# A branch prefetch hint at the top of TensorE's loop over rounds

## The chip, the cores and the metric

The kernel runs on one core of one Trainium2 chip. The metric is the device time of one execution in microseconds. Three executions of the kernel before gave 1239.11, 1243.03 and 1248.18 us, so the median is 1243.03 us.

## The reference

The inputs are float32: `x` of 4 x 4096 x 192, `weight_gen` of 4 x 4096 x 8 x 7, `w_in` of 192 x 2048 and `w_out` of 2048 x 192. What is computed is a dynamic causal convolution over seven taps, followed by a gated two-layer product on all 16384 tokens:

```python
w = exp(weight_gen - max(weight_gen, axis=-1))        # softmax over the 7 taps
w = w / (sum(w, axis=-1) + 1e-09)
out = einsum('bshk,bskhg->bshg', w, x_unf)            # x_unf: the 7 latest tokens, zeros before the start
x = out.reshape(16384, 192)
h = x @ w_in
g = h * clip(h + 3.0, 0.0, 6.0) / 6.0
return g @ w_out
```

## The kernel before, in words

The work is cut into 16 rounds (`PAIRS`) of 1024 tokens. A round has two halves of 512 tokens. GpSimd computes the convolution of each half (`attend`), TensorE transposes it, and then 16 tiles of 128 hidden columns are filled: TensorE computes `h` of a tile into one of four PSUM banks (`work`), ScalarE takes relu(h + 3) (L261), VectorE multiplies (L357), ScalarE rounds the product to the type that the matmuls read (`g_hi`, L266), VectorE stores what the rounding lost (`g_lo`, L362), and TensorE multiplies both parts by `w_out` into four PSUM banks `sums` (L548 and L551). The float32 precision is kept by products of such high and low parts, which is why there are many matmuls per tile.

TensorE works on two tiles at a time, a duo. In a round there are 18 duos, 16 of tiles and 2 of transposes. One duo is: a wait until VectorE has left the banks (`bank_free`), the first half of the fill (L512 and L513), a few products of earlier tiles, the second half of the fill (L526 and L527), and products again. The Python loop over the 18 duos is written out, and only the loop over rounds is a loop on the chip. It runs 15 times on TensorE, and the sixteenth round is written out behind it. So one iteration is one long piece of straight code: 856 matmuls, each with its weight load, and 88 instructions that count registers, wait or branch, 1800 in all. Its last instruction is a compare-and-branch back to its first. The branch is taken 14 times; the fifteenth time it falls through to the last round.

The other engines have loops over rounds of their own (SyncE, GpSimd, ScalarE and VectorE), each far shorter than TensorE's: 14 rows of instructions on SyncE, 47 on GpSimd, 121 on ScalarE and 136 on VectorE. The engines meet only through semaphores, and the order of work on each is written out by hand in the program; no scheduler moves anything.

All instructions that the loop itself makes (the register of the round, its increase, and the branch) have the line of the `with` statement, L586. The first matmul of an iteration is that of L512 for duo 3, the last ones are L548 and L551 of duo 20.

Of the kernel before, what the change touches and what calls it, by code (L numbers as in the profile page):

```python
# [26 lines left out]
PAIRS = S // (RUNS * TOKENS)  # L27
# [419 lines left out]
def tensor_program(nc, pe, t, s):  # L447
# [110 lines left out]
    def duo(q, d, last=False):  # L558
        bank_free(q, 2 * d - 3, last)
        fill_first(q, d, last)  # L560
        starts = d % HALF_DUOS == FIRST_DUO
        multiply(q, parts_after(d, 0), 1, None if starts else turns_before(q, d, 0), by_sets=starts)
        fill_second(q, d, last)
        multiply(q, parts_after(d, 1), 0, turns_before(q, d, 1))
# [18 lines left out]
    multiply(0, parts_after(FIRST_DUO, 1), 0, 2)  # L583
    pe.wait_ge(s.w_out_lo, 2)

    with pe.Fori(0, PAIRS - 1) as q:  # L586
        for d in range(FIRST_DUO + 1, FIRST_DUO + 1 + DUOS):
            duo(q, d)
    for d in range(FIRST_DUO + 1, DUOS + 2):
# [89 lines left out]
def build(nc, *arrays):  # L679
    with ExitStack() as ctx:  # L680
        dram = Dram(*arrays)
        t = Buffers(lambda name, shape, dt=F32: ctx.enter_context(nc.sbuf_tensor(name, shape, dt)),
                    lambda name, shape: ctx.enter_context(nc.psum_tensor(name, shape, F32)))
        s = Semaphores(lambda name: ctx.enter_context(nc.semaphore(name)))
        block = ctx.enter_context(nc.Block())

        @block.sync
        def _(sp):
            sync_program(nc, sp, dram, t, s)

        @block.gpsimd
        def _(pool):
            gpsimd_program(nc, pool, t, s)

        @block.scalar
        def _(act):
            scalar_program(nc, act, dram, t, s)

        @block.vector
        def _(dve):  # L700
            vector_program(nc, dve, t, s)

        @block.tensor
        def _(pe):
            tensor_program(nc, pe, t, s)
# [17 lines left out]
```

## Time and profile before

| | |
|---|---|
| median of three executions | 1243.03 us |
| profiled execution | 1239.38 us |
| its span, from the first to the last instruction | 1236.6 us |
| mean granted TensorE clock | 0.985 of full speed |
| TensorE busy with matmuls | 1170.4 us, 95% of the span |
| VectorE, ScalarE, GpSimd busy | 66%, 54%, 56% |
| instruction fetches (queue q8) | 139 packets, 2.28 MB |

### The profile page before, as it was taken

To read this page: it belongs to the slowest core of one execution; us is meant where nothing else is said; L and a number is where in the kernel's file an instruction comes from. 1 tells how busy PE (TensorE), PEld (TensorE's weight loads), DVE (VectorE), ACT (ScalarE), POOL (GpSimd) and SP (SyncE) were. 2 spreads that over 40 slices of the span, in tenths; PEclk is the share of its full clock that TensorE was granted. 3 is DMA by queue.
4 is the path that set the end of the run, shared out by engine and by line. 5 is a ranking of instruction groups with operands and counts; after the bars stand their busy time and mean duration, and the time that the engine had idled before them with its cause. 6 is when DMAs were issued, how large, how long until landed. Compare 5 with 4: busy or idle time off the path is not lost.

```text
span 1236.6 us, 33823 instructions
## 1 busy us (share of the span) xinstructions
PE 1170.4 (95%) x13696; PEld 1095.7 (89%) x13696; DVE 818.9 (66%) x1362; ACT 662.4 (54%) x1269; POOL 691.1 (56%) x455
## 2 busy tenths in 40 slices
PE   1999999999999999999999999999999999999998
PEld 1898998989989898998989989899898989989997
DVE  7866766657666666666667666676666666666664
ACT  3554555545555455455555555555454555555553
POOL 7793671927639085490936719276390854909300
PEclk9999999999999999999999999999999999999999
DMA  6101010010100101001010100101001010010000
GB/s 177 46 22 59 20 48 15 22 60 21 47 15 22 60 22 59 2 29 52 22 60 16 52 15 22 60 22 58 3 22 60 22 59 2 27 54 14 15 15 14
DMA packets 12203, 44.25 MB, mean 36 GB/s; under 512 B 1183, under 2 KB 5279, under 8 KB 10139
## 3 DMA queue, kind: packets, MB, share of 16 engines
q1 hardware_dynamic: 12059, 41.93, 9.7%
q8 instruction: 139, 2.28, 0.8%
q14 instruction: 5, 0.04, 0.0%
HBM read 29.34 MB, written 12.58 MB: 34 GB/s over the span
## 4 chain that ended last, share of the span: by engine, by line
PE 92%; DVE 3%; ACT 2%; issue 1%; POOL 1%; DMA 0%; DVEq 0%; ACTq 0%
PE sums L548 32%; PE work L512 16%; PE work L526 13%; PE sums L551 13%; PE work L527 9%; PE work L513 7%; DVE g_lo L362 2%; DVE work L357 1%; ACT g_hi L266 1%; ACT relu L261 1%; PE work L477 1%; PE work L464 1%; POOL pool_acc L166 0%; POOL pool_prod L164 0%; DVE w_in L413 0%
## 5 line engine op out<-in xcount | busy, mean ns | idle before, releaser
L548 PE MATMUL sums<-w_out,g_hi 64*128 64x384 f32 x4096 | 649.7, 357 | 2.8 <-DVE g_lo L362 2.1
L551 PE MATMUL sums<-w_out,g_lo 64*128 64x192 f32 x4096 | 558.4, 249 | 0.0
L357 DVE SCALAR_TENSOR_TENSOR work<-relu,work 128x512 f32<-128x512 f32 x512 | 331.2, 693 | 331.1 <-ACT relu L261 329.8
L261 ACT ACTIVATE relu<-work 128x512 f32<-128x512 f32 x512 | 279.4, 601 | 400.6 <-PE work L527 398.2
L548 PEld LDWEIGHTS sums<-w_out,g_hi 64*128 64x128 f32 x4096 | 438.4, 186 | 19.8 <-issue 3.1
L551 PEld LDWEIGHTS sums<-w_out,g_lo 64*128 64x128 f32 x4096 | 442.9, 189 | 0.2
L266 ACT CAST g_hi<-work 128x512 fp32r<-128x512 f32 x512 | 300.9, 588 | 76.0 <-DVE work L357 73.6
L362 DVE TENSOR_TENSOR g_lo<-work,g_hi 128x512 fp32r<-128x512 f32 x512 | 330.1, 687 | 14.4
L159 POOL TENSOR_TENSOR pool_acc<-x_in,w_soft 128x768 f32<-128x768 f32 (+1 forms) x32 | 50.0, 1562 | 461.4 <-DVE w_soft L351 454.6
L166 POOL TENSOR_TENSOR pool_acc<-pool_acc,pool_prod 128x768 f32<-128x768 f32 (+1 forms) x160 | 295.6, 1847 | 0.0
L512 PE MATMUL work<-xt_a,w_in 64*128 64x512 f32 x768 | 235.7, 414 | 35.9 <-DVE g_lo L362 28.1
L164 POOL TENSOR_TENSOR pool_prod<-x_in,w_soft 128x768 f32<-128x768 f32 (+1 forms) x160 | 248.6, 1554 | 0.0
L513 PE MATMUL work<-xt_a,w_in 64*128 64x512 f32 x768 | 235.4, 413 | 0.0
L526 PE MATMUL work<-xt_a,w_in 64*128 64x512 f32 x768 | 226.8, 401 | 0.0
L527 PE MATMUL work<-xt_a,w_in 64*128 64x512 f32 x768 | 226.4, 401 | 0.0
L512 PEld LDWEIGHTS work<-xt_a,w_in 64*128 64x128 f32 x768 | 126.1, 190 | 51.0 <-DVE g_lo L362 33.5
L512 PE MATMUL work<-xt_b,w_in 64*128 64x512 f32 (+1 forms) x512 | 133.0, 340 | 0.0
L513 PE MATMUL work<-xt_b,w_in 64*128 64x512 f32 (+1 forms) x512 | 132.9, 340 | 0.0
L526 PE MATMUL work<-xt_b,w_in 64*128 64x512 f32 (+1 forms) x512 | 129.3, 332 | 0.0
L527 PE MATMUL work<-xt_b,w_in 64*128 64x512 f32 (+1 forms) x512 | 129.2, 332 | 0.0
L526 PEld LDWEIGHTS work<-xt_a,w_in 64*128 64x128 f32 x768 | 124.1, 187 | 5.4
L513 PEld LDWEIGHTS work<-xt_a,w_in 64*128 64x128 f32 x768 | 126.2, 190 | 1.4
(47 smaller groups left out, 960.4 us busy)
## 6 DMA issues: line engine op xcount, KB each, us to landing
x_in<-x_dram SPq DMA_DIRECT2D x15, 1344.0 KB, 6.0
out_dram<-out_stage SPq DMA_DIRECT2D x32, 384.0 KB, 3.0
w_raw<-weight_gen_dram SPq DMA_DIRECT2D x16, 224.0 KB, 3.0
w_out_raw<-moe_w_out_dram SPq DMA_DIRECT2D x1, 1152.0 KB, 13.3
x_in<-x_dram SPq DMA_DIRECT2D x1, 768.0 KB, 5.0
w_in_raw<-moe_w_in_dram SPq DMA_DIRECT2D x1, 768.0 KB, 8.1
w_in_raw<-moe_w_in_dram SPq DMA_DIRECT2D x2, 384.0 KB, 10.1
w_out_raw<-moe_w_out_dram SPq DMA_DIRECT2D x1, 384.0 KB, 6.2
```

The lines of the kernel that those rows point to most:

```text
L164: eng.tensor_tensor(prod[k % 3], x_tap(k), w_tap(k), ALU.mult).then_inc(step, 1)
L166: eng.tensor_tensor(acc, acc, prod[(k - 1) % 3], ALU.add).then_inc(step, 1)
L261: nc.scalar.activation(t.relu[:, m % 2, :], t.work[m % BANKS][:], ACT.Relu, bias=3.0).then_inc(s.relu_ready, 1)
L266: nc.scalar.copy(t.g_hi[:, m % G_SLOTS, :], t.work[m % BANKS][:]).then_inc(s.g_hi_ready, 1)
L357: nc.vector.scalar_tensor_tensor(bank[:], t.relu[:, m % 2, :], 6.0, bank[:], ALU.min, ALU.mult).then_inc(s.gated, 1)
L362: nc.vector.tensor_tensor(t.g_lo[:, m % G_SLOTS, :], t.work[m % BANKS][:], f32(t.g_hi[:, m % G_SLOTS, :]), ALU.subtract).then_inc(s.g_lo_r ...
L512: nc.tensor.matmul(*upper, start=(i == 0), stop=False)
L513: ins = nc.tensor.matmul(*lower, start=(i == 0), stop=False)
L526: ins_upper = nc.tensor.matmul(*upper, start=False, stop=(i == len(both) - 1))
L527: ins_lower = nc.tensor.matmul(*lower, start=False, stop=(i == len(both) - 1))
L548: nc.tensor.matmul(t.sums[n][:, 0:2 * D], t.g_hi[rows, m % G_SLOTS, n * P:(n + 1) * P], t.w_out[rows, j, :], start=(j == 0 and part == 0), ...
L551: ins = nc.tensor.matmul(t.sums[n][:, D:2 * D], t.g_lo[rows, m % G_SLOTS, n * P:(n + 1) * P], t.w_out[rows, j, 0:D], start=False, stop=las ...
```

## The change

One line is different. The loop over rounds on TensorE is opened by the general form, for that engine alone, with the option `hint_back_edge`:

```diff
-    with pe.Fori(0, PAIRS - 1) as q:
+    with nc.Fori(0, PAIRS - 1, engines=[mybir.EngineType.PE], hint_back_edge=True) as q:
         for d in range(FIRST_DUO + 1, FIRST_DUO + 1 + DUOS):
             duo(q, d)
```

In the program this adds one instruction to TensorE's stream. It stands first in the loop's body, so it is executed in each of the 15 iterations, and it names the compare-and-branch at the end of the body, with the outcome "likely taken". The piece of the difference on TensorE at the loop's entry, behind the products ahead of the loop:

```order
 L551 MATMUL sums<-w_out,g_lo 128x192 x2
 L586 UNCONDITIONAL_BRANCH
+L586 BRANCH_PREFETCH_HINT
 L586 ISA
 L512 MATMUL work<-xt_a,w_in 128x512
```

The unconditional branch leads into the loop, the hint is new, and the row "ISA" is the register work that was the first instruction of the body before. The other end of the body, on TensorE too, reads as before:

```order
L551 MATMUL sums2<-w_out,g_lo 128x192
L551 MATMUL sums3<-w_out,g_lo 128x192
L586 REGISTER_ALU
L586 COMPARE_AND_BRANCH
L512 MATMUL work2<-xt_a,w_in 128x512
L513 MATMUL work3<-xt_a,w_in 128x512
```

The compare-and-branch is the instruction that the hint names. The matmuls behind it are the first of the sixteenth round. Nothing is moved, and the other four engines' programs are the same.

## Rows read from the trace of the kernel before

**Rows 1.** The page: span, busy times, queue of instruction fetches (packets, MB, share).
```profile
span 1236.6 us, 33823 instructions
PE 1170.4 (95%) x13696; PEld 1095.7 (89%) x13696; DVE 818.9 (66%) x1362; ACT 662.4 (54%) x1269; POOL 691.1 (56%) x455
q8 instruction: 139, 2.28, 0.8%
```

**Rows 2.** Waits of PE, whole span: us in total, times, longest us.
```profile
PE work L512 <- DVE g_lo L362: 28.1, 12, 2.6
PE work L463 <- POOL attn_b L170: 22.9, 1, 22.9
PE work L512 <- issue: 5.4, 2, 2.7
PE work L512 <- DVE xt_b L371: 2.4, 1, 2.4
PE sums L548 <- DVE g_lo L362: 2.1, 1, 2.1
```

**Rows 3.** Stretches between two iterations: window, us, busy per engine, PEclk, DMA share, GB/s.
```profile
114.68:117.42 2.74, 0.00 (x1) 0.01 (x1) 2.65 (x5) 0.92 (x2) 0.00 (x0) 1.00 0.02 7
...
342.33:344.33 2.00, 0.01 (x1) 0.01 (x1) 1.95 (x4) 0.91 (x2) 0.00 (x0) 1.00 0.00 0
...
1091.92:1094.59 2.67, 0.01 (x2) 0.01 (x1) 2.58 (x5) 0.90 (x2) 0.00 (x0) 0.99 0.02 7
sum 33.46, PE 0.04 PEld 0.09 DVE 32.27 ACT 12.66 POOL 0.00; mean PE 0.00 PEld 0.01 DVE 2.31 ACT 0.90 POOL 0.00
```

**Rows 4.** Instructions of L586: count, ns least/median/most, first and last start.
```profile
L586 PEldq FUSED_REGOPS  x15: 50/50/53, 41.7 to 1094.5; - x15
L586 PEldq COMPARE_BRANCH  x15: 83/3582/4007, 113.2 to 1166.6; - x15
```

**Rows 5.** Same columns: iterations at full clock, six in all, first and last.
```profile
42.75:114.68 71.93, 71.92 (x860) 66.38 (x856) 50.58 (x85) 41.15 (x80) 52.20 (x35) 1.00 0.15 54
...
1019.92:1091.92 72.00, 72.00 (x856) 67.71 (x856) 47.48 (x82) 39.99 (x78) 43.14 (x28) 1.00 0.10 35
sum 431.33, PE 431.31 PEld 403.52 DVE 287.88 ACT 241.13 POOL 267.85; mean PE 71.88 PEld 67.25 DVE 47.98 ACT 40.19 POOL 44.64
```

**Rows 6.** Same columns: eight iterations partly at lower clock, first and last.
```profile
117.42:190.71 73.29, 73.28 (x856) 68.04 (x856) 46.94 (x81) 40.01 (x78) 43.12 (x28) 0.98 0.10 35
...
944.78:1017.78 73.00, 73.00 (x856) 68.65 (x856) 47.33 (x81) 40.02 (x78) 43.12 (x28) 0.98 0.10 35
sum 587.05, PE 587.02 PEld 548.87 DVE 377.53 ACT 320.01 POOL 345.02; mean PE 73.38 PEld 68.61 DVE 47.19 ACT 40.00 POOL 43.13
```

**Rows 7.** Same columns: the fifteenth iteration's stretch.
```profile
1094.59:1166.50 71.91, 71.91 (x838) 68.17 (x840) 45.50 (x79) 38.75 (x76) 43.15 (x28) 0.98 0.03 12
```

**Rows 8.** Timeline of DVE, at the loop's entry and at one edge: start, us.
```profile
40.84 1.29 DVE L362 TENSOR_TENSOR g_lo<-work,g_hi 128x512 fp32r<-128x512 f32 x2
...
188.38 1.29 DVE L362 TENSOR_TENSOR g_lo<-work,g_hi 128x512 fp32r<-128x512 f32 x2
189.70 1.29 DVE L357 SCALAR_TENSOR_TENSOR work<-relu,work 128x512 f32<-128x512 f32 x2
191.05 1.29 DVE L362 TENSOR_TENSOR g_lo<-work,g_hi 128x512 fp32r<-128x512 f32 x2
```

**Rows 9.** DMA over 192.91:268.63, one iteration with its edge: packets, MB.
```profile
q8 instruction: 9, 0.15, 0.9%
```

**Rows 10.** DMA over 186:194 in 40 slices of 0.2 us: GB/s, fetch packets.
```profile
GB/s 0 0 0 0 0 0 0 0 0 0 0 82 215 399 399 338 399 108 0 15 97 15 31 31 0 0 0 0 0 0 0 0 0 0 0 0 0 0 0 82
q8 instruction: 3, 0.05, 2.5%
```

## The prediction

> **What bounds the kernel now.** I read the page first. The span is 1236.6 us and TensorE is busy for 1170.4 us of it, 95%; the next engine, VectorE, has 818.9 us [rows 1]. So TensorE sets the time, and only its idle time and its speed can change. Next I read its waits [rows 2]. One of 22.9 us is the start, before the first transposes. The rest is nearly all one group: before L512, 28.1 us in 12 waits and 5.4 us in 2 waits, 14 waits of up to 2.7 us each. Fourteen is the number of times the loop over rounds goes back to its top. The stretches between iterations show that these waits are all there: 14 of them, 33.46 us in sum, 2.39 us each, with TensorE at nothing and GpSimd at nothing [rows 3].
>
> The view puts 12 of these waits down to VectorE's `g_lo`. That must be checked, because a hint to the branch can't help a wait for data. Across the edge from 190.71 to 192.91 us, VectorE ends a pair of `g_lo` at 188.38 + 1.29 = 189.67 us and the next pair only at 192.34 us [rows 8]. The fill at the top of an iteration writes the banks of two duos earlier, so it needs the first pair, and that was over 3.2 us before TensorE went on and 1.0 us before it stopped. The later pair is what `g_lo` happened to end in the gap. What did hold TensorE stands in the rows of L586: the compare-and-branch took 83 ns at its shortest, which is the one that fell through, and 3582 ns in the median and 4007 ns at most [rows 4]. A taken branch is thus some 3.5 us dearer than one not taken. The sequencer reaches it ahead of the matmuls: the first branch starts at about 113.2 us [rows 4], the last matmul ends at 114.68 us [rows 3]. So about 1.4 us of it is covered, and the remainder is the gap.
>
> What the branch does in that time is seen in the instruction queue. One iteration fetches 9 packets of about 16 KB (0.15 MB) [rows 9], and the whole run 139 [rows 1]. Around one edge, a single packet in a slice of 0.2 us reads as 82 GB/s: one at 188.2 to 188.4 us, one at 190.0 to 190.2 us (97, with 15 of other traffic) and one at 193.8 to 194.0 us [rows 10]. The branch was reached shortly before the second. I read this as follows: the first packet is the code behind the branch, fetched in advance and not used; the second is the top of the loop, fetched only when the branch asks for it; the third is the block after it.
>
> Last, the clock. Six iterations ran wholly at the granted clock of 1.00 (2.4 GHz) and took 71.88 us in the mean (431.33 / 6) [rows 5]. Eight show a mean of 0.98, part of them at the lower level, and took 73.38 us (587.05 / 8) [rows 6]; the fifteenth shows 0.98 too [rows 7]. The first iteration was entered without an edge and has 1.00. Of the 14 behind a gap nine show 0.98 and five 1.00. I read the fall as something that a gap brings about in some cases: 1.50 us each.
>
> **The change, part by part.** It adds one instruction at the top of the body and names the branch at its end as likely taken. Nothing else moves.
>
> *The gaps.* If the top of the loop is at hand when the branch is taken, the branch costs what the untaken one does, 83 ns, which lies within the 1.4 us by which the sequencer is ahead. Then the whole 33.5 us goes.
>
> *The clock.* Without gaps, the nine iterations at 73.38 us become like the six at 71.88 us: 9 x 1.50 = 13.5 us. The lower end of this term is 0 (the clock falls for another reason), the upper 13.5 us. I take 13.5, since the only iteration without a gap before it had none.
>
> *What is late next.* The gap let the other engines catch up, so their margin must be looked at. The first iteration has none of it: VectorE's pair of `g_lo` ends at 40.84 + 1.29 = 42.13 us [rows 8], and the first fill starts at 42.75 us [rows 5]. That is 0.6 us of margin, and that iteration took 71.93 us with the softmax work of the next round in it, no longer than the others at full clock. No wait takes the gap's place. GpSimd works 43 to 52 us in an iteration of 72 us [rows 5], ScalarE 40, VectorE 48.
>
> *The hint itself.* No row shows one. The nearest are the 50 ns of the register operation beside it and the 83 ns of the untaken branch [rows 4]. Hidden behind the queued matmuls it costs 0; fully exposed, 15 x 0.083 = 1.2 us. I take 0, because the sequencer is ahead at this place.
>
> *The exit.* The fifteenth time the branch falls through. If the hint brings the top of the loop in place of the code behind the branch, that code is missing once, when the sixteenth round comes to it. Bounds: 0, or one gap with the lower clock behind it, 2.4 + 1.5 = 3.9 us. I take 2.4.
>
> *Sum.* Against the profiled execution's 1239.4 us: 1239.4 - 33.5 - 13.5 + 2.4 = 1194.8 us. The profiled execution stands at the lower end of the three runs (1239.1 to 1248.2), 3.7 us under their median of 1243.0. Between 9 and 14 edges with the lower clock lie 7.5 us, which could be that spread, and it would go with the edges; a part may stay. I put the median after at 1196 us.
>
> *A rule against it.* The rows show that a body of 1800 instructions is fetched anew in each iteration [rows 9]. The Trainium skill ("Runtime: NRT & Kernel Launch", "Instruction fetch mechanics") says that TensorE's instruction memory is 128 KiB, or 2048 instructions, and in a note just below that it is only two lines and that prefetch is purely sequential, a taken branch out of the two lines forcing a fetch. By the 2048 instructions alone this body would fit and the edges would be free, so the trace speaks against that figure as it stands, unless the packet fetched past the branch pushes the top out. By "purely sequential" a hint could do nothing, and the sum would be 1239.4 us.
>
> **The rivals.**
>
> *A, the forecast: no gap is left.* The top of the loop is at hand at the branch. 1190 to 1199 us. Chance 0.46.
>
> *B: the fetch starts earlier, but not early enough.* The hint turns the first packet of the edge into the top of the loop. It starts 1.8 us before the one that the branch asks for now [rows 10]. Of 2.39 us, 0.6 us are left, 14 x 0.6 = 8.3 us. With no fall of the clock that gives 1194.8 + 8.3 = 1203 us; with all nine, 1216.6 us. For it speaks that in the trace of before every iteration fetches all its blocks, one at a time and just ahead of their use; against it, that one block fewer may let the whole body stay. Chance 0.33. The Trainium skill's note on two lines, on the same page, would make this case the rule, since the top lies seven lines back at the branch.
>
> *C: the hint does nothing.* Prefetching stays sequential, the branch still asks for its own target, and the time is that of before plus at most 1.2 us: 1239 to 1244 us. For it speaks that the trace of before shows sequential fetches alone. Chance 0.14. The skill's "purely sequential" is this case.
>
 The gain per iteration is (33.5 + 13.5) / 15 = 3.1 us, so one such block takes back most of it and from the second on the kernel is slower: with two 1192.4 + 15 x 2 x 2.4 = 1264 us, with all seven 1444 us. Nothing in the profile speaks for or against it. Chance 0.07.
>
> **How the numbers follow.** The predicted time is A's, 1196 us. A and B hold 0.79 and reach from 1190 us (no cost at the exit, and a little less of the rest) to 1216 us (B with the clock's falls kept), which is the range. A measurement of this kernel can tell about 1% from no change, 12 us; A and B are faster by more, 0.79; C is within it, 0.14; D is slower, 0.07.
>
> **What would show it.** In the changed kernel's profile, under A the compare-and-branch at L586 has a median near the 83 ns, the waits of L512 are gone, every iteration from the second takes about 71.9 us with a PEclk of 1.00, and the nine packets per iteration become eight or fewer; if the body stays in the memory, the run's packets fall from 139 to some 20. Under B the branch takes about 1.7 us and 14 short gaps remain, with eight packets per iteration. Under C the rows of L586 are as before, under D waits "issue" appear within the iterations. A branch that is short while gaps remain at the top would prove me wrong on VectorE: then the `g_lo` wait was real.

## The result, and the profile after

The changed kernel takes 1187.8 us in the median of four runs (1186.15 to 1189.66), against 1244.03 us of the kernel before in the runs beside it (1239.11 to 1248.18). The ratio is 0.955 with an interval of 0.9511 to 0.9588. The direction and the mechanism were those of case A, but the time lies 2.2 us under the lower end of the range (1190 us), so the range missed it. The profiled execution took 1187.49 us, 51.9 us less than that of before.

The page of the changed kernel, its span, busy times and instruction fetches:

```profile
span 1185.5 us, 33838 instructions
PE 1151.4 (97%) x13696; PEld 1070.8 (90%) x13696; DVE 818.9 (69%) x1362; ACT 662.0 (56%) x1269; POOL 690.7 (58%) x455
q8 instruction: 13, 0.21, 0.1%
```

Against [rows 1], the other engines' busy times are the same and the fetches fell from 139 packets to 13. Seven of the 13 packets come before 102 us, in the first iteration, and the next one only at 1116.6 us. So the loop's body is fetched once and then stays. Next the waits of PE in the changed kernel (us in total, times, longest), all of them:

```profile
PE work L463 <- POOL attn_b L170: 23.1, 1, 23.1
PE sums L548 <- DVE g_lo L362: 3.3, 2, 2.5
PE work L512 <- DVE xt_b L371: 2.4, 1, 2.4
PE sums L548 <- PE sums L551: 0.5, 3, 0.2
```

The 14 waits at L512 of [rows 2] are gone, also the 12 that were put down to VectorE's `g_lo`. Had they been waits for data, a hint to the branch would not have removed them. The instructions of L586 in the changed kernel (count, ns least/median/most, first and last start):

```profile
L586 PEldq BRANCH_PREFETCH_HINT  x15: 31/31/45, 41.9 to 1044.0; - x15
L586 PEldq FUSED_REGOPS  x15: 50/50/50, 42.0 to 1044.1; - x15
L586 PEldq COMPARE_BRANCH  x15: 80/216/257, 112.9 to 1115.5; - x15
```

A taken branch now takes 216 ns, not 3582 ns [rows 4], and the hint 31 ns. (The prediction had the taken branch at the 83 ns of the untaken one; both lie within the 1.4 us by which the sequencer is ahead, so nothing comes of it.) The timeline of PE in the changed kernel, across the first edge (start, us):

```profile
113.99 0.36 PE L548 MATMUL sums<-w_out,g_hi 64*128 64x384 f32 x2
114.19 0.25 PE L551 MATMUL sums<-w_out,g_lo 64*128 64x192 f32 x2
114.28 0.42 PE L512 MATMUL work<-xt_a,w_in 64*128 64x512 f32 x1
114.28 0.42 PE L513 MATMUL work<-xt_a,w_in 64*128 64x512 f32 x1
```

The next iteration's first matmuls start 0.09 us after the last one's start, as anywhere else in the stream; the last one still runs to 114.44 us. This overlap matters for the sum below.

The whole loop in one window, from the first matmul of the first iteration to the first matmul of the sixteenth round, and what follows to the end. The kernel before:

```profile
42.75:1167.83 1125.08, 1091.61 (x12844) 1021.98 (x12842) 744.48 (x1261) 613.61 (x1186) 656.01 (x427) 0.99 0.10 34
1167.83:1236.60 68.77, 63.64 (x748) 60.18 (x744) 39.21 (x66) 33.63 (x65) 0.00 (x0) 0.98 0.04 13
```

and the changed one:

```profile
42.44:1116.85 1074.41, 1074.41 (x12845) 1000.78 (x12842) 744.97 (x1262) 613.48 (x1187) 656.08 (x427) 1.00 0.09 33
1116.85:1185.50 68.65, 63.55 (x748) 58.38 (x744) 39.15 (x66) 33.54 (x65) 0.00 (x0) 0.98 0.03 13
```

The loop is 50.67 us shorter, the part ahead of it 0.31 us, the last round 0.12 us. That is the 51.1 us between the spans. Outside the span lie 0.8 us more (1239.4 - 1236.6 = 2.8 before, 1187.5 - 1185.5 = 2.0 now). An iteration takes 1074.41 / 15 = 71.63 us from start to start, TensorE is busy in all of it, and the clock is 1.00.

### The profile page after: what moved, and what is told of

It reads as the page before. It is cut to its first block, busy times and chain, and to the rows that moved or that the text cites. A ratio compares the mean times of both kernels' runs of the same rounds, so it can differ in the third digit from the quotient of the medians.

```text
span 1185.5 us, 33838 instructions
## 1 busy us (share of the span) xinstructions
PE 1151.4 (97%) x13696; PEld 1070.8 (90%) x13696; DVE 818.9 (69%) x1362; ACT 662.0 (56%) x1269; POOL 690.7 (58%) x455
## 4 chain that ended last, share of the span: by engine, by line
PE 96%; DVE 2%; POOL 1%; issue 0%; DMA 0%; ACT 0%; DVEq 0%; ACTq 0%
PE sums L548 34%; PE work L512 16%; PE sums L551 15%; PE work L526 14%; PE work L527 9%; PE work L513 7%; PE work L477 1%; PE work L464 0%; DVE w_out L419 0%; POOL pool_acc L166 0%; POOL pool_prod L164 0%; DVE w_in L413 0%; DMA w_raw<-weight_gen_dram 0%; PE work L463 0%; DVE g_lo L362 0%
## 5 line engine op out<-in xcount | busy, mean ns | idle before, releaser
L548 PE MATMUL sums<-w_out,g_hi 64*128 64x384 f32 x4096 | 631.0, 354 | 3.9 <-DVE g_lo L362 3.3
L551 PE MATMUL sums<-w_out,g_lo 64*128 64x192 f32 x4096 | 536.1, 247 | 0.0
L548 PEld LDWEIGHTS sums<-w_out,g_hi 64*128 64x128 f32 x4096 | 410.2, 184 | 23.3 <-issue 3.5
L551 PEld LDWEIGHTS sums<-w_out,g_lo 64*128 64x128 f32 x4096 | 415.7, 187 | 0.0
L512 PE MATMUL work<-xt_a,w_in 64*128 64x512 f32 x768 | 229.2, 404 | 2.4 <-DVE xt_b L371 2.4
L513 PE MATMUL work<-xt_a,w_in 64*128 64x512 f32 x768 | 229.1, 404 | 0.0
L526 PE MATMUL work<-xt_a,w_in 64*128 64x512 f32 x768 | 226.2, 400 | 0.0
L527 PE MATMUL work<-xt_a,w_in 64*128 64x512 f32 x768 | 226.1, 400 | 0.0
L512 PEld LDWEIGHTS work<-xt_a,w_in 64*128 64x128 f32 x768 | 123.6, 186 | 15.0 <-DVE g_lo L362 5.1
L512 PE MATMUL work<-xt_b,w_in 64*128 64x512 f32 (+1 forms) x512 | 129.8, 333 | 0.0
L513 PE MATMUL work<-xt_b,w_in 64*128 64x512 f32 (+1 forms) x512 | 129.7, 333 | 0.0
L526 PE MATMUL work<-xt_b,w_in 64*128 64x512 f32 (+1 forms) x512 | 129.0, 331 | 0.0
L527 PE MATMUL work<-xt_b,w_in 64*128 64x512 f32 (+1 forms) x512 | 129.0, 331 | 0.0
L526 PEld LDWEIGHTS work<-xt_a,w_in 64*128 64x128 f32 x768 | 123.3, 186 | 6.1
L527 PEld LDWEIGHTS work<-xt_a,w_in 64*128 64x128 f32 x768 | 123.3, 186 | 3.0
```

Source lines behind the costliest of these rows:

```text
L512: nc.tensor.matmul(*upper, start=(i == 0), stop=False)
L513: ins = nc.tensor.matmul(*lower, start=(i == 0), stop=False)
L526: ins_upper = nc.tensor.matmul(*upper, start=False, stop=(i == len(both) - 1))
L527: ins_lower = nc.tensor.matmul(*lower, start=False, stop=(i == len(both) - 1))
L548: nc.tensor.matmul(t.sums[n][:, 0:2 * D], t.g_hi[rows, m % G_SLOTS, n * P:(n + 1) * P], t.w_out[rows, j, :], start=(j == 0 and part == 0), ...
L551: ins = nc.tensor.matmul(t.sums[n][:, D:2 * D], t.g_lo[rows, m % G_SLOTS, n * P:(n + 1) * P], t.w_out[rows, j, 0:D], start=False, stop=las ...
```

## Experiments

The predicted rival B (an earlier fetch of the top) and the forecast A (nothing to fetch) are told apart by the packets above. Two questions were open: why the body stays, and what the lower clock hangs on. The trace suggests an answer to the first. Before, each iteration of 1800 instructions fetched nine packets of 16 KB, and one of them was the block past the branch, so the body lay in eight. Nothing was left of the top when the branch asked for it. The Trainium skill ("Advanced Engine Details and Errata", "ISA Cache") gives 256 instructions for such a block; by the runs below the tipping point agrees with that. Theory R is that TensorE's instruction memory holds eight blocks, and that the hint's effect is that this ninth block is not fetched. Rival S is that it is the hint itself that makes a far branch cheap.

**No hint, a body that lies in seven blocks or in eight.** Two kernels with the same instructions and no hint. To make the body small enough, each of the four tiles of two duos is filled without its fifth product (8 matmuls of 856 are left out); the loop's first instruction is put at place 0 or place 100 of a block.

```diff
+    def terms(d):
+        return 4 if d in (4, 5) else 5
...
-        for i, (upper, lower) in enumerate(zip(products(2 * d, 0), products(2 * d + 1, 1))):
+        for i, (upper, lower) in enumerate(zip(products(2 * d, 0)[:terms(d)], products(2 * d + 1, 1))):
...
-    with nc.Fori(0, PAIRS - 1, engines=[mybir.EngineType.PE], hint_back_edge=True) as q:
+    with nc.Fori(0, PAIRS - 1, engines=[mybir.EngineType.PE], hint_back_edge=False,
+                 head_slot={mybir.EngineType.PE: 0}) as q:
```

> No hint. Two of the 16 duos of tiles in each round fill without their fifth product, which leaves 8 matmuls of 856 out, so one iteration is 1784 instructions in place of 1800; the loop's first instruction is put at the first place of a fetched block of 256. The body then lies in 7 blocks, 8 with the one fetched past the branch. Theory R (the hint helps because the unused block behind the branch is not fetched any more, so that the whole body stays in TensorE's instruction memory, which holds 8 blocks): no gap at any edge though there is no hint, COMPARE_BRANCH about 0.2 us, some 13 to 15 instruction packets in the run, time about 1180 us (1187.8 less 16 x 0.5 us for the matmuls left out). Theory S (the hint is needed, because a taken branch far back always asks for its block again): 14 gaps of about 2.4 us, branch 3.5 us, some 125 packets, 1231 to 1238 us.

> The same instructions as the kernel whose loop starts at the first place of a block, with the same 8 matmuls of 856 left out and no hint, but the loop starts at place 100 of a block. It lies in 8 blocks, 9 with the one behind the branch. Theory R: one block too many, so every block is fetched again in each iteration: 14 gaps of about 2.4 us, 9 packets per iteration, about 139 in all, 1231 to 1238 us, some 50 us above the run with the same work. Theory S: the same as that run, whatever it gives.

Measured, one run each: 1179.09 us with the top at place 0, 1236.79 us at place 100, beside 1241.59 us of the kernel before. L589 is the loop's line here. The branch (ns least/median/most), and from the page the fetches, with the top at place 0:

```profile
L589 PEldq COMPARE_BRANCH  x16: 76/208/1495, 41.9 to 1107.8; - x16
```
```profile
q8 instruction: 14, 0.23, 0.1%
```

and the same two views with the top at place 100:

```profile
L589 PEldq COMPARE_BRANCH  x16: 83/3546/3857, 41.7 to 1164.8; - x16
```
```profile
q8 instruction: 139, 2.28, 0.7%
```

and its waits at the top:

```profile
PE work L515 <- DVE g_lo L362: 32.8, 14, 2.6
```

This decides for R. The same instructions, moved by 100 places, are 57.7 us apart, and without any hint the branch takes 0.21 us where the body and the block behind it make eight. S expected the two to be equal. (The 1495 ns are one branch at 41.9 us, the entry into the loop, which is there because of the placement.)

**Where the hint has to stand.** The loop is written out by hand, with the hint directly ahead of the closing two instructions or ahead of duo 19. Both kernels in one cut, each has one of the two marked pieces:

```diff
+        for d in range(FIRST_DUO + 1, FIRST_DUO + 1 + DUOS):
+            if d == 19:                                   # second kernel
+                place = pe.mark_branch_hint_location()
+            duo(q, d)
+        place = pe.mark_branch_hint_location()            # first kernel
+        nc.regs_alu(registers, registers, 1, op=ALU.add)
+        pe.br_lt(registers, PAIRS - 1, on_true="rounds_loop", on_false="rounds_end").branch_hint(place)
```

> All work done. The hint stands not at the top of the iteration but directly ahead of the loop's closing two instructions, 1800 instructions later, inside the block that holds the branch. If the hint acts only by steering the advance fetch that is made when the branch's block is entered (theory R), it comes too late, since that fetch is already under way: gaps of 2 to 2.6 us and about 139 packets, 1238 to 1246 us. If it makes a fetch or keeps the body by itself at whatever place it is executed (theory T), the gaps are gone or much shorter: 1188 to 1205 us.

> All work done. The hint stands ahead of duo 19, the last but one of the iteration, some 230 instructions ahead of the branch and in the block before the branch's. Theory R: as good as at the top, no gaps, 13 packets, 1186 to 1190 us. A theory by which it must be known for the whole iteration (U) gives gaps of up to 2.4 us and over 100 packets, 1200 to 1244 us.

Measured, one run each: 1251.26 us with the hint last, 5 us above the top of the expected range, and 1189.50 us with the hint ahead of duo 19. The hint, the branch, and the page's line on fetches, with the hint last:

```profile
L596 PEldq BRANCH_PREFETCH_HINT  x15: 41/41/41, 112.6 to 1179.0; - x15
```
```profile
L598 PEldq COMPARE_BRANCH  x15: 88/3578/4001, 112.8 to 1179.2; - x15
```
```profile
q8 instruction: 140, 2.29, 0.8%
```

and the same with the hint ahead of duo 19:

```profile
L594 PEldq BRANCH_PREFETCH_HINT  x15: 31/31/45, 104.1 to 1108.5; - x15
```
```profile
L598 PEldq COMPARE_BRANCH  x15: 80/216/257, 113.2 to 1117.7; - x15
```
```profile
q8 instruction: 14, 0.23, 0.1%
```

Nine microseconds ahead of the branch it does all that it does at the top, so it need not be known for the whole iteration (theory U falls). 0.2 us ahead it does nothing: in that run the packet past the branch starts at 111.8 us and the hint at 112.6 us, so that block is already on its way (theory T falls). The two kernels have the same instructions in another order, so it is neither the added instruction nor the other form of the loop that helps. These two runs alone would also fit a hint that needs some lead; the placements in nine blocks below speak for the steering of that one advance fetch. The single run of 1251.26 us was above the kernel before, and the same kernel was then timed against that one:

> All work done, the hint directly ahead of the loop's closing two instructions; timed against the kernel before. The single run of it had the old gaps and 18 stretches of half clock in place of 10. If a late hint is simply useless, the ratio to before is 0.995 to 1.005. If it costs something, 1.005 to 1.01.

Measured: 1241.35 us in the median of 10 runs against 1242.44 us of 19, a ratio of 0.9998 (0.998 to 1.0017). A late hint is useless, and no cost of it shows within 0.2%. The lines of the core in three executions, whose gaps in the loop sum to 34.7, 36.1 and 33.5 us, show where the 1251 us came from (span, mean granted clock): the kernel with the late hint, twice, and the kernel before.

```profile
core 0: 1249.5 us, clock 0.974
```
```profile
core 0: 1243.0 us, clock 0.980
```
```profile
core 0: 1236.6 us, clock 0.985
```

From 0.985 to 0.974 the time lost to the lower clock grows by an estimated 0.026 x 1249.5 - 0.015 x 1236.6 = 13.9 us, and the spans are 12.9 us apart. In the run of 1251 us the lower clock came at all 14 edges and lasted twice as long at four of them; in the kernel before it came at 9. This differs between runs of one kernel too: of the 19 runs of the kernel before, the fastest (1235.38 us) had a mean clock of 0.987 and the slowest (1244.74 us) 0.979. The 0.008 between them are an estimated 10 us, and the times are 9.4 us apart.

**A body of eight blocks or of nine, with the hint.** All work is done. Eleven increments of semaphores that nobody reads stand behind each duo. The body is then 1999 instructions long with the hint, the same in four kernels; only the place of its first instruction differs.

```diff
+    with nc.Fori(0, PAIRS - 1, engines=[mybir.EngineType.PE], hint_back_edge=True,
+                 head_slot={mybir.EngineType.PE: 30}) as q:     # 30, 50, 239, 128
         for d in range(FIRST_DUO + 1, FIRST_DUO + 1 + DUOS):
             duo(q, d)
+            for i in range(11):
+                pe.sem_inc(s.pad[i % 6], 1)
```

> All work done, hint at the top. Behind each duo stand 11 increments of semaphores that nobody reads, 198 per iteration, which makes the body 1999 instructions; the loop starts at place 30 of a block, so the body still ends in its eighth block (30 + 1999 = 2029 of 2048). Theory R (eight blocks stay): no gaps, branch 0.22 us, 13 or 14 packets, 1186 to 1192 us plus what the increments cost where the sequencer is not ahead. If they cost their 51 ns each on the path it would be 15 x 198 x 0.051 = 151 us more; I expect under 10 us, since they are spread over the duos.

> The same instructions as the kernel with the padded body in eight blocks, but the loop starts at place 50, so its branch is the very first instruction of a ninth block (50 + 1998 = 2048). Theory R: nine blocks do not stay, 9 packets per iteration, about 139 in all; the hint steers a fetch that starts only as the branch is reached, so gaps of 2 to 2.6 us, some 50 us above the eight-block run. Theory V (a hint makes the top available whatever the size of the body, by fetching it well ahead): no gaps.

> The same instructions once more, loop at place 239: the branch lies at place 189 of the ninth block (239 + 1998 = 2237). Nine packets per iteration again, but the block of the branch is entered some 7 us before the branch, more than the 3.5 us that a fetch at the branch cost. Theory R with the fetch steered on entering the block (case B of the prediction with time enough): no gaps, the time of the eight-block run, about 135 packets. If the hint only helps where the body stays: 14 gaps of 2.4 us.

> The padded instructions once more with the hint at the top (1999 per iteration), loop at place 128: nine blocks, the branch at place 78 of the ninth, and 128 instructions between the loop's first and the next block. The two other placements in nine blocks had a stall before the top (branch at place 0) or 3 us behind it (top at place 239). If one fetch at a time, each begun when a block is entered, explains both, then here both fetches are in time: about 135 packets, a branch below 1 us, no gap of over 1 us at or just behind the top, and 1277 to 1290 us, like the eight-block run. If a body that does not stay always stalls somewhere, 1325 to 1350 us.

| top at place | blocks | time, one run | branch, median | packets |
|---|---|---|---|---|
| 30 | 8 | 1277.46 us | 228 ns | 15 |
| 50, branch first in the ninth | 9 | 1348.08 us | 3344 ns | 140 |
| 239, branch at 189 of the ninth | 9 | 1329.90 us | 360 ns | 142 |
| 128, branch at 78 of the ninth | 9 | 1279.90 us | 446 ns | 141 |

The increments themselves cost 90 us against the changed kernel (1277.5 - 1187.5), where I had expected under 10: that expectation was wrong, and the comparison holds among these four alone. Twenty places further on, the body no longer stays: from 15 packets to 140, and 70.6 us more, where about 50 were expected. Eight blocks of 256 is where it tips (30 + 1999 = 2029, 50 + 1999 = 2049). The hint stood a whole iteration ahead of the branch here, and yet the packet of the top started only 1.0 us behind the branch's start, because the branch is the first instruction of its block (theory V falls). The gaps are 3.7 to 4.2 us and not 2 to 2.6: the sequencer reached this branch only as TensorE ran dry, without its lead of 1.4 us.

The kernel with its top at place 239 was expected to be as fast as the first and is not. Its timeline of PE behind one edge (start, us, idle before):

```profile
200.79 0.26 PE L551 MATMUL sums<-w_out,g_lo 64*128 64x192 f32 x2
201.82 0.49 PE L512 MATMUL work<-xt_a,w_in 64*128 64x512 f32 x1 [0.77 <-issue]
...
204.91 0.49 PE L513 MATMUL work<-xt_b,w_in 64*128 64x512 f32 x1 [1.92 <-issue]
```

and in its waits of PE there are 14 of these, 1.9 us in the mean:

```profile
PE work L513 <- issue: 26.4, 14, 2.2
```

The branch is short, but a stall ends 3 us behind the top's first matmul. The top has 17 instructions left in its own block, and the block after it is fetched only when the branch arrives at the top (its packet starts 1.1 us behind the branch's start). The stall was moved from ahead of the top to behind it. The 52.4 us over the first kernel are these 26.4 us and some 20 us of lower clock (estimated from the mean clocks, 0.983 x 1328.1 us against 0.998 x 1275.6 us); the rest was not traced.

With 128 places left, and the branch 78 places into its block, both fetches are in time. The DMA of that kernel over 192 to 200 us, in slices of 0.2 us, around the branch at 197.9 us:

```profile
GB/s 0 0 0 0 0 0 0 0 0 0 0 0 0 82 0 184 384 399 353 399 123 15 0 15 15 15 31 31 0 0 0 0 0 0 0 82 0 0 0 0
q8 instruction: 2, 0.03, 2.0%
```

The packet of the top starts 3.1 us ahead of the branch, that of the next block 1.2 us behind it; with the branch at place 189 the first starts 7.8 us ahead, with the branch at place 0 not ahead at all. So the advance fetch is tied to the entry into the branch's block, and the hint turns it to the top. 141 packets are fetched, and the kernel takes 1279.9 us all the same, 2.4 us more than the first. The earlier fetch of the top that case B of the prediction assumed exists, then, but with a body of nine blocks and not of eight.

**A gap without any fetch.** The changed kernel with increments of unread semaphores ahead of the branch, 70 of them and then 22, body in eight blocks.

```diff
             duo(q, d)
+        for i in range(22):                # 70 in the first of the two
+            pe.sem_inc(s.pad[i % 6], 1)
```

> All work done, hint at the top, body in eight blocks, so no fetches. 70 increments of unread semaphores stand directly ahead of the loop's closing instructions, 70 x 0.051 = 3.6 us of the sequencer's time, about what the taken branch took before. It makes 15 gaps of about 2.2 us with nothing fetched. If an idle TensorE alone brings the lower clock: some 7 to 14 stretches at half clock after the gaps and 1188 + 15 x 2.2 + 10 x 1.5 = about 1236 us. If the clock fell for the fetches or something else of the old edge: the clock stays at 1.00 and the time is about 1221 us.

> All work done, hint at the top, body in eight blocks, nothing fetched after the first iteration. 22 increments of unread semaphores directly ahead of the branch. By the run with 70 of them, where the gaps were 9.8 us, one costs (9.8 + 1.4) / 70 = 0.16 us of the sequencer, so 22 give 3.5 us, what the taken branch took before, and gaps of about 2.2 us with the sequencer's lead of 1.4 us. If an idle time of that length alone brings the lower clock, 7 to 14 of the 15 gaps are followed by a stretch at half clock and the time is 1188 + 15 x 2.3 + 10 x 1.5 = 1237 us; if it needs the fetches, the clock stays at 1.00 and the time is about 1222 us.

With 70 of them: 1366.83 us where about 1236 were expected, 15 packets, and gaps of 9.8 us and not 2.2. One increment shows 51 ns in the trace and costs the sequencer (9.8 + 1.4) / 70 = 0.16 us. The clock fell at every gap, but the gaps are four times those of before, so only the second kernel compares. With 22: 1242.66 us in the median of 10 runs, a ratio to the kernel before of 1.0016 (0.9992 to 1.004). Its waits and fetches, and two of its gaps with the iteration between them (window, us, busy per engine, PEclk, DMA share, GB/s):

```profile
PE work L512 <- DVE g_lo L362: 35.9, 15, 2.5
```
```profile
q8 instruction: 15, 0.25, 0.1%
```
```profile
115.16:117.62 2.46, 0.01 (x2) 0.01 (x2) 2.37 (x5) 0.92 (x2) 0.00 (x0) 1.00 0.00 0
117.62:190.81 73.19, 73.19 (x856) 69.16 (x856) 47.20 (x81) 39.99 (x78) 43.14 (x28) 0.98 0.09 33
190.81:193.23 2.42, 0.01 (x2) 0.01 (x2) 2.33 (x5) 0.93 (x2) 0.00 (x0) 0.92 0.00 0
```

Nothing is fetched inside the loop after its first iteration, the gaps are as long as before, and the iteration is 73.19 us at a mean clock of 0.98, as in [rows 6]; the clock fell at 11 of the 15 gaps. So the idle time alone brings the lower clock, and the fetches are not needed for it. It also repeats the false reading of [rows 2]: these waits too are put down to `g_lo`, although what makes them is known here.

No version of the whole computation faster than the changed kernel was found: with the hint TensorE is busy in all of the loop, and the experiments with less time left work out.

## Why the prediction missed its range

The steps that failed are terms of the sum, not the mechanism: the gaps were taken as 33.5 us and gave back 36.0, with 1.2 us more of open cause, and the exit was taken as 2.4 us and cost nothing. Neither alone would have carried the time under 1190 us; together, and with smaller errors on the same side, they did, since the low end of the range lay too close to the sum.

*What bounds the kernel, and what the gaps are*: right. The argument that the waits put down to VectorE's `g_lo` are no waits for it held, and no wait took the place of the gap. The part on "what is late next" held too.

*The gaps*, 33.5 us: the first of two terms that were mis-sized. A stretch from the last matmul's end to the next one's start leaves out that without a gap the two overlap. In the changed kernel the last matmul ends at 114.44 us and the next starts at 114.28 us, 0.16 us earlier; over the 14 edges this is 0.16 to 0.21 us each, 2.5 us in sum. The term is 36 us.

*The clock*, 13.5 us: its cause was shown by the 22 increments, and its size follows from [rows 5, 6]. The clock in the loop is 1.00 now. The loop's 50.67 us are thus 33.5 (gaps) + 2.5 (overlap) + 13.5 (clock), and 1.2 us that remain, 0.08 us per iteration. Where iterations at full clock are laid side by side, the first ten matmuls behind a gap lose 0.07 us, and the iteration's second half loses some more. Its cause wasn't tried and stays open.

*The exit*, 2.4 us: the second term that was mis-sized. It costs nothing. The last round takes 68.65 us against 68.77 us. The DMA of the changed kernel over 1112 to 1120 us, in slices of 0.2 us, shows the fetch that this takes:

```profile
GB/s 0 0 0 0 0 0 0 0 0 0 0 0 154 445 353 430 415 169 0 0 0 0 0 82 0 41 0 0 0 0 0 0 0 0 0 0 0 0 0 0
q8 instruction: 1, 0.02, 0.8%
```

The 82 GB/s at 1116.6 us are the packet behind the branch, 1.1 us after the fall-through at 1115.5 us. It isn't needed at once, because of where the branch lies in its block. The trace of before shows no places, but the run with the top at place 100 gives a measure: its branch is at place 91 of its block (100 + 1783 - 1792), and the packet past it starts 1.0 us ahead of it. Before, the unused packet started 0.9 us ahead of the branch [rows 10]. So the branch lies, by estimate, at some place near 90, and about 165 instructions were still to come when the fetch began. The kernel of 1999 instructions with its top at place 30 shows the other case. Its branch is at place 236, with 19 places left, and its only stall of that length in the loop or behind it stands there, in the last round (start, us, idle before):

```profile
1205.32 0.27 PE L512 MATMUL work<-xt_b,w_in 64*128 64x256 f32 x1
1207.75 0.28 PE L513 MATMUL work<-xt_b,w_in 64*128 64x256 f32 x1 [2.16 <-issue]
```

So what I feared exists, 2.2 us where the branch lies near the end of its block, and nothing where it does not. My bounds were 0 and 3.9 us. That the unused packet starts so shortly ahead of the branch, while the packets of an iteration are some 10 us apart, would have let me take the lower.

*Start and outside*: 0.3 us and 0.8 us, no term of mine.

*The hint itself*, taken as 0: a row of 31 ns, nothing visible on the path.

*The median*: I added 1.2 us for a part of the spread of before that might stay. The spread went from 9.1 us to 3.5 us, and the median after lies 0.3 us above the profiled execution. The runs of the kernel before show that its spread hangs on how often the clock falls. The median shows none of it any more.

Together: 1194.8 - 2.4 (exit) - 2.5 (overlap) - 1.2 (pace) - 0.3 - 0.8 = 1187.6 us, against 1187.5 us in the profiled execution. *The range*: I set its low end at 1190 us as "no cost at the exit, and a little less of the rest". With the exit at 0 the sum was 1192.4 us, and 2.4 us were left for the errors of all other terms. That was too narrow on this side; on the other side there were 20 us.

*The rule against it.* The Trainium skill ("Runtime: NRT & Kernel Launch", "Instruction fetch mechanics") gives TensorE 2048 instructions, and the runs with 2029 and 2049 places agree with it. Its note that the memory is "only 2 cache lines" disagrees with them, since the body of eight blocks stays, and its "Prefetch is purely sequential" does not hold once a hint is given: 13 packets in place of 139, and with nine blocks the packet of the top ahead of the branch. The prediction named the right reading, that the packet past the branch pushes the top out, as a possibility only, and gave A a chance of 0.46.

*Rival D*: the hint given at the top cost no advance fetch on the way. In the changed kernel nothing had to be fetched; in the three kernels of nine blocks nine packets came per iteration, and between the top and the branch TensorE waits twice per iteration, 0.8 to 1.0 us each, as in the kernel of eight blocks, which fetches nothing there (the kernel with its top at place 239 has the stall at its second block besides).

## What to carry to other kernels

A loop with a long body can pay for its branch in two ways, by the time the branch takes and by the clock after the gap; count the fetch packets per iteration first. If they show the whole body fetched anew although it would just fit, the one block past the branch is the first suspect. Here a hint removed all of it, and so did 16 instructions fewer with the top at the start of a block. A wait that the profile puts down to a data semaphore must be checked against the time at which the needed value was ready.

## What the runs showed of the hardware

- TensorE's instruction memory keeps eight blocks of 16 KB: a body that ends at place 2029 is fetched once (15 packets), the same body ending at place 2049 in every iteration (140 packets).
- The sequencer fetches one block ahead when it enters a block: in the kernels of nine blocks the packet starts 7.8 us ahead of a branch at place 189, some 3 us ahead of one at place 78, and 1.0 us behind the start of one at place 0. A hint 0.2 us ahead of the branch was too late, one 9 us ahead was in time. Where the top has only 17 places left in its block, the next block is late by 1.9 us in the mean.
- An increment of a semaphore on TensorE's sequencer shows 51 ns in the trace and costs 0.16 us of its time; 198 of them spread over an iteration made it 5.8 us longer (77.4 us against 71.6).
- Where a loop falls through with 19 places left in its block, the last round stalled for 2.2 us; with an estimated 165 left it did not.
- Idle times of 2.0 to 2.7 us brought the lower clock at 9 of 14 edges in the profile of before, at 1.5 us each, and idle times of 2.0 to 2.6 us at 14 of 14 in the run with the top at place 100. How often it comes differs between runs of the same kernel, by some 9 us in total in the 19 runs of the kernel before. In the kernel of 1999 instructions in eight blocks, idle times of 0.5 to 0.9 us, about three in an iteration, brought none.
